# A fused attention and two-expert-layer kernel: identity transposes on TensorE while it waits, and its expert loops aligned to a fetch block

## The chip, the cores and the metric

The kernel runs on one core of one Trainium2 chip. The metric is the device time of one execution in microseconds (us); lower is better. Nothing is shared with other cores.

## What is computed

Three stages follow each other. A linear recurrence with a complex decay (4 batches, 8 heads, 768 steps, head size 48) gives 3072 rows of 384 numbers. A first expert layer sends every row to one of 8 experts (384 to 1024 to 384, with a ReLU between) and scales it by a gate. A second one does the same for the rows whose skip score is positive, and adds the result to them.

```
for t in range(S):
    new_re = ar * S_re - ai * S_im
    new_im = ar * S_im + ai * S_re
    S_re, S_im = (new_re + kv, new_im)
    y[:, :, t] = einsum('bhd,bhde->bhe', q[:, :, t], S_re)
...
expert_idx = argmax(logits, axis=1)
for e in range(E):
    mask = expert_idx == e
    h = maximum(x[mask] @ w1[e], 0.0)
    out[mask] = gate_w[mask, None] * (h @ w2[e])
```

## The kernel before

The recurrence is worked in 6 blocks c of 128 steps for 4 batches b, 24 steps n in all. For each block the logarithms of the decay are summed over its 128 steps by a matmul with a triangle of ones (`log_sum`, L1576, source tile `lm`), and its angles likewise (`angle_sum`, L1588 for block 0, source tile `an`). Exponentials of the first sums (tiles `ep` and `em`, ScalarE) and sines of the second (`kk`, `turn`, `cs`) are multiplied into q and k; TensorE transposes the products (L1619), and scores (L1633), state (L1650) and outputs (L1667, L1668) follow.

Both expert layers m = 0 and 1 share code. Rows are sorted by expert with a list in DRAM: GpSimd writes row numbers to it, reads the numbers of a tile back (`members`, L595, tile `idx_g`, semaphore `s_list[m]`) and gathers the rows with four indirect DMAs (`gather`, L602, tile `xg`, semaphore `s_xg[m]`). A tile s has up to 512 rows of one expert. On TensorE `rows_in` (L1776) transposes the tile, ScalarE and VectorE split it into a high and a low part (`xh` L930, `xl` L1359), `up` does 72 matmuls (L1788 to L1790), `down_a` or `down_b` the second product (L1805 to L1807, L1821 to L1823) and `results` L1835. `up` begins when `xl` is complete.

The tile count `used` and the length class of each tile (`code`, two bits a tile, looked up by `by_length`) are known at run time only. So each engine runs an outer loop over s in steps of 2, with an inner loop over the two halves, and each part of a tile's work stands four times, once for each length, behind compares and branches. `rows_in` for tile s + 1 stands inside the body of tile s, between the first part of the second product and its rest. Synchronisation is by semaphores written out by hand; the order on each engine is the order of the code. TensorE's instructions are written once in the order in which they run, apart from these branches; every matmul in the listings below is a weight load and a matmul, two instructions (four where the operands are plain float32 and it is no transpose, which runs in two passes).

Of the kernel before, what the change touches and what calls it, by code (L numbers as in the profile page):

```python
# [22 lines left out]
P = 128  # L23
# [4 lines left out]
def build(nc, H, a, qk, v, emb, tau, w1_a, w2_a, w_skip, w_gate, w1_b, w2_b, out):  # L28
    B, S, HD = v.shape
    D = HD // H  # L30
    C = S // P
    E, _, F = w1_a.shape
    N = B * S
    NT = N // P
    NS = N // 512 + E - 1
# [26 lines left out]
    with keep:  # L62
        def tensors(stack):
            return lambda name, shape, dt=F32: stack.enter_context(nc.sbuf_tensor(name, shape, dt))

        def sem(name):
            return keep.enter_context(nc.semaphore(name))
# [7 lines left out]
        ident = const("ident", [P, P])  # L75
# [74 lines left out]
        t_ = tensors(att)  # L150
# [34 lines left out]
        t_ = tensors(moe)  # L185
# [17 lines left out]
        T = [bank[0], bank[1]]  # L203
# [6 lines left out]
        DN = [bank[3], bank[4]]  # L210
# [13 lines left out]
        s_lm = sem("s_lm")  # L224
# [57 lines left out]
        def layer(name):  # L282
            return [sem(f"{name}_{m}") for m in range(2)]
# [12 lines left out]
        s_list = layer("s_list")  # L296
# [53 lines left out]
        def sum_bank(c, b):  # L350

            return (PL, PT[0], PT[1], PY)[b] if c == 0 else PL
# [1204 lines left out]
        def _(pe):  # L1557
            t = nc.tensor
# [8 lines left out]
            def log_sum(c, b):  # L1567

                n = B * c + b
                to = sum_bank(c, b)[:, 0:HD]  # L1570
                if c:
                    pe.wait_ge(s_exp, n)
                if b == 0 and c in (1, 2):
                    pe.wait_ge(s_turn, n)
                pe.wait_ge(s_logs, b // 2 + 1 if c == 0 else 2 * c + 2)
                t.matmul(to, tri_half[:, :], lm[:, b, :], start=True, stop=True).then_inc(s_L, 1)  # L1576

            def angle_sum(c, b):

                n = B * c + b  # L1580
                to = turn_bank(c, b)[:, 0:HD]
                if c == 0:
                    if b == 1:
                        pe.wait_ge(s_exp, 1)
                    if b == 3:
                        pe.wait_ge(s_turn, 1)
                    pe.wait_ge(s_angle, b // 2 + 1)
                    t.matmul(to, tri_turn[:, :], an[:, b, :], start=True, stop=True).then_inc(s_TH, 1)  # L1588
                else:
                    pe.wait_ge(s_turn, n - 1 if c == 1 and b > 1 else B * c if c == 1 else n)  # L1590
                    if c == 1 and b == 1:
                        pe.wait_ge(s_exp, 2 * B)
                    if c == 1:
                        pe.wait_ge(s_angle, 2 * c + 2)
                        t.matmul(to, tri_turn[:, :], an[:, b, :], start=True, stop=False)
                        t.matmul(to, last_row[:, :], turn[:, b, :], start=False, stop=True).then_inc(s_TH, 1)
                    else:
                        pe.wait_ge(s_carry, c - 1)
                        t.matmul(to, tri_turn[:, :], an[:, b, :], start=True, stop=True).then_inc(s_TH, 1)

            def sums(c, b):

                log_sum(c, b)
                angle_sum(c, b)
# [87 lines left out]
            def step(n):  # L1692
# [42 lines left out]
                if second and b == 0:  # L1735
                    sums(c + 1, 1)

            for b in range(B):
                log_sum(0, b)
            for b in range(B):  # L1740
                angle_sum(0, b)
            for n in range(2):
# [11 lines left out]
            for m in range(2):  # L1754
                tab = tab_of[m]

                def tiles(n):
                    return [(j, min(P, n - j * P)) for j in range((n + P - 1) // P)]

                def by_length(s, part):  # L1760
                    for i, n in enumerate(SIZES[m]):
                        with pe.If(((code >> (s * 2)) & 3) == i):
                            part(n)

                def rows_in(s, par):

                    pe.wait_ge(s_xg[m], s * 64 + 64)
                    if not isinstance(s, int):
                        pe.wait_ge(s_hl[m], FC * s)

                    def parts(n):
                        for side in (0,) if isinstance(s, int) else (0, 1):
                            with pe.If(par == side):
                                for k_ in range(KC):
                                    for j, w in tiles(n):
                                        i = t.transpose(U[k_][:, j * P:j * P + w], xg[0:w, side, j, k_ * P:(k_ + 1) * P], ident[0:w, 0:w])  # L1776
                                    i.then_inc(s_xT[m], 1)
                    by_length(s, parts)
# [59 lines left out]
                def rank_next(s):  # L1838

                    four = [P, TJ, E]  # L1840
                    to = QR.rearrange("p (t e) -> p t e", e=E)
                    pe.wait_ge(s_ohb, s + 1)
                    pe.wait_ge(s_sumb, s + 1)
                    t.matmul(to, before_t[:, :], oh_b[:, :, :], start=True, stop=False)
                    for j in range(1, TJ):
                        t.matmul(to[:, j:TJ, :], minus[:, :], oh_b[:, 0:TJ - j, :], start=False, stop=False)
                    t.matmul(to, minus[:, :], sum_b[:, :].unsqueeze(1).to_broadcast(four), start=False, stop=False)
                    t.matmul(to, minus[:, :], starts[:, :].unsqueeze(1).to_broadcast(four), start=False, stop=True).then_inc(s_rankb, 1)

                def count_next():  # L1850
                    for j in range(TJ):
                        t.matmul(QC, minus[:, :], oh_b[:, j, :], start=j == 0, stop=False)
                    t.matmul(QC, minus[:, :], sum_b[:, :], start=False, stop=True).then_inc(s_count, 1)

                def main(s, par):

                    pe.wait_ge(s_w1l[m], s + 1)
                    pe.wait_ge(s_xl[m], KC * s + KC)
                    by_length(s, lambda n: up(s, n))
                    if m == 0:  # L1860
                        with pe.If(s > 0):
                            rank_next(s - 1)
                        by_length(s, lambda n: down_a(s, n, (0,)))
                    else:
                        down_b(s, 0, P, False)
                    with pe.If(used > s + 1):
                        rows_in(s + 1, 1 - par)
                    if m == 0:
                        def rest(n):
                            down_a(s, n, (1, 2))  # L1870
                            results(s, n)
                    else:
                        def rest(n):
                            for j, w in tiles(n)[1:]:
                                down_b(s, j, w, j == tiles(n)[-1][0])
                    by_length(s, rest)
# [3 lines left out]
                pe.wait_ge(s_tab, m + 1)  # L1880
                used = pe.value_load(tab[0:1, USED:USED + 1], min_val=E, max_val=NS)
                code = pe.snap(pe.value_load(tab[0:1, CODE:CODE + 1], min_val=0, max_val=16383) + (pe.value_load(tab[0:1, CODE + 1:CODE + 2], min_val=0, max_val=16383) << 14))
                rows_in(0, 0)
                with pe.Fori(0, NS + 1, 2) as t_:
                    with pe.Fori(0, 2) as par:
                        s = t_ + par
                        with pe.If(used > s):
                            main(s, par)
                        if m == 0:
                            with pe.If(used == s):  # L1890
                                rank_next(s - 1)
                                count_next()
# [24 lines left out]
```

## Time and profile before

| | |
|---|---|
| times of the runs shown | 799.91, 801.9, 809.33 us; median 801.9 us |
| profiled execution | 801.38 us, its span 799.8 us |
| TensorE busy with matmuls | 663.7 us, 83% of the span |
| VectorE, ScalarE, GpSimd busy | 495.0, 406.6, 281.9 us |
| mean granted TensorE clock | 0.922 of full |

The span is from the first to the last instruction of the profiled execution; 1.6 us of that execution's time lie around it. The granted clock is 1.00 for 2.4 GHz and 0.50 for 1.2 GHz; in a stretch with both it is the mean. The attention stage lasts to about 312 us, the first expert layer from 330 to 600 us, the second from 626 us to the end.

### The profile page before, as it was taken

What the parts mean: (1) busy time and instruction counts of PE and PEld (TensorE: products, weight loads), DVE (VectorE), ACT (ScalarE), POOL (GpSimd) and SP (SyncE); (2) the same over time, 40 slices, a digit from 0 to 9 for tenths busy, and PEclk for the clock granted to TensorE, in tenths of its full rate; (3) what the DMA queues carried; (4) which work ended last, traced back from release to release, by engine and by line L of the source; (5) the groups of instructions that cost most, each with busy time, mean ns of one, the idle gap of its engine ahead of it and who ended that gap; (6) DMA issues with size and microseconds to landing.
All of it is one profiled execution on the core that took longest, in us unless ns stands there. A gap on an engine that the chain in (4) does not pass through costs nothing.

```text
span 799.8 us, 15830 instructions
## 1 busy us (share of the span) xinstructions
PE 663.7 (83%) x4754; PEld 608.9 (76%) x4754; DVE 495.0 (62%) x1169; ACT 406.6 (51%) x747; POOL 281.9 (35%) x315
## 2 busy tenths in 40 slices
PE   0678878998989993389999999999980689999993
PEld 0377767888878883378998999999870589999992
DVE  5564684977888665164755746757535366677770
ACT  7675586786685631162634635545421345455550
POOL 4304113142333232504335354262115425255531
PEclk9889789997999996599999999999995699999997
DMA  7431441524132520424335334353221255555630
GB/s 263 123 124 47 120 160 41 161 82 134 68 84 81 167 96 22 141 83 139 88 131 187 103 133 142 110 195 110 78 79 40 99 181 185 176 202 183 204 100 20
DMA packets 68580, 97.61 MB, mean 122 GB/s; under 512 B 28194, under 2 KB 51244, under 8 KB 68524
## 3 DMA queue, kind: packets, MB, share of 16 engines
q1 hardware_dynamic: 58028, 82.06, 31.8%
q0 software_dynamic: 10496, 14.84, 5.7%
q8 instruction: 30, 0.49, 0.2%
q14 instruction: 26, 0.21, 0.1%
HBM read 86.79 MB, written 21.04 MB: 135 GB/s over the span
## 4 chain that ended last, share of the span: by engine, by line
PE 70%; DVE 9%; ACT 8%; issue 8%; DMA 3%; POOL 1%; POOLq 0%; SPq 0%; DVEq 0%; ACTq 0%
PE bank L1788 8%; PE bank L1790 8%; PE bank L1789 8%; PE bank L1805 5%; PE bank L1807 4%; PE bank L1806 4%; PE bank L1619 3%; PE bank L1821 3%; PE bank L1633 3%; PE bank L1823 3%; PE bank L1822 3%; PE bank L1835 3%; PE bank L1650 3%; PE bank L1576 2%; PE bank L1776 2%
## 5 line engine op out<-in xcount | busy, mean ns | idle before, releaser
L1788 PE MATMUL bank<-xh,w1h 128*128 128x256 f32 (+3 forms) x384 | 124.7, 325 | 11.8 <-issue 5.7
L938 ACT ACTIVATE hh<-bank 128x256 fp32r<-128x256 f32 (+3 forms) x128 | 57.7, 451 | 135.6 <-PE bank L1790 135.3
L1789 PE MATMUL bank<-xh,w1l 128*128 128x256 f32 (+3 forms) x384 | 123.1, 321 | 0.0
L1790 PE MATMUL bank<-xl,w1h 128*128 128x256 f32 (+3 forms) x384 | 123.1, 320 | 0.0
L1367 DVE SCALAR_TENSOR_TENSOR hl<-bank,hh 128x256 fp32r<-128x256 f32 (+3 forms) x128 | 64.9, 507 | 61.1 <-ACT hh L938 53.6
L620 POOL DMA_INDIRECT out<-yg,idx_o x64 | 68.8, 1075 | 80.0 <-DVE yg L1428 47.7
L1788 PEld LDWEIGHTS bank<-xh,w1h 128*128 128x128 f32 x384 | 74.4, 194 | 16.9 <-issue 15.8
L1789 PEld LDWEIGHTS bank<-xh,w1l 128*128 128x128 f32 x384 | 74.3, 194 | 1.0
L1790 PEld LDWEIGHTS bank<-xl,w1h 128*128 128x128 f32 x384 | 74.2, 193 | 1.1
L1200 DVE TENSOR_TENSOR w2l<-raw,w2h 128x384 fp32r<-128x384 f32 x128 | 71.0, 555 | 0.0
L548 POOL TENSOR_TENSOR qk_t<-qk_t,ep 128x384 f32<-128x384 f32 x24 | 25.6, 1067 | 128.3 <-ACT em L750 101.5
L1805 PE MATMUL bank<-hh,w2h 128*128 128x384 f32 (+1 forms) x192 | 68.4, 356 | 1.5 <-issue 1.2
L1807 PE MATMUL bank<-hl,w2h 128*128 128x384 f32 (+1 forms) x192 | 67.1, 349 | 0.0
L1806 PE MATMUL bank<-hh,w2l 128*128 128x384 f32 (+1 forms) x192 | 67.0, 349 | 0.0
L631 POOL DMA_INDIRECT list<-pay,idx_b x32 | 37.0, 1156 | 83.3 <-DVE pay L1496 61.4
L801 ACT ACTIVATE w2h<-raw 128x384 fp32r<-128x384 f32 x128 | 66.2, 517 | 0.0
L1200 DVE TENSOR_TENSOR w1l<-raw,w1h 128x1024 fp32r<-128x1024 f32 x48 | 58.4, 1223 | 8.4 <-issue 6.6
L1776 PE MATMUL bank<-ident,xg 128*128 128x128 f32 (+1 forms) x132 | 21.3, 294 | 48.0 <-DMA xg<-out,idx_g 26.3
L602 POOL DMA_INDIRECT xg<-out,idx_g x32 | 33.6, 1051 | 71.2 <-DVE yg L1450 51.6
L556 POOL DMA_INDIRECT list<-token,idx_a x24 | 25.3, 1053 | 94.5 <-DVE idx_a L1178 77.4
L1776 PEld LDWEIGHTS bank<-ident,xg 128*128 128x128 f32 (+1 forms) x132 | 16.7, 150 | 51.7 <-issue 50.7
L930 ACT ACTIVATE xh<-bank 128x256 fp32r<-128x256 f32 (+3 forms) x48 | 19.5, 451 | 71.7 <-PE bank L1776 70.4
(230 smaller groups left out, 1655.0 us busy)
## 6 DMA issues: line engine op xcount, KB each, us to landing
raw<-in_moe_w SPq DMA_DIRECT2D x32, 1536.0 KB, 7.0
a_t<-in_a SPq DMA_DIRECT2D x24, 384.0 KB, 4.8
qk_t<-in_qk SPq DMA_DIRECT2D x24, 384.0 KB, 3.4
x_a<-ysb SPq DMA_DIRECT2D x24, 196.0 KB, 1.9
vt<-in_v SPq DMA_DIRECT2D x24, 192.0 KB, 3.5
list<-nobody SPq DMA_DIRECT2D x2, 1536.0 KB, 8.4
out<-yg,idx_o POOLq DMA_INDIRECT x64, 2.6
xg<-x_a,idx_g POOLq DMA_INDIRECT x32, 5.5
```

The source lines that it names most:

```text
L620: g.indirect_dma_start(out, bass.IndirectOffsetOnAxis(idx_o[:, par, j:j + 1], 0), yg[:, par, j, :], None, bounds_check=N - 1, oob_is_err=F ...
L801: return a_.activation(hi[:, at], raw[:, at], ACT.Copy)
L938: a_.activation(hh[:, f, 0:n], U[f % 3][:, 0:n], ACT.Relu).then_inc(s_hh[m], 1)
L1200: return d.tensor_tensor(lo[:, at], raw[:, at], hi[:, at].bitcast(F32), ALU.subtract)
L1367: d.scalar_tensor_tensor(out=hl[:, f, 0:n], in0=U[f % 3][:, 0:n], scalar=0.0, in1=hh[:, f, 0:n].bitcast(F32), op0=ALU.max, op1=ALU.subtrac ...
L1776: i = t.transpose(U[k_][:, j * P:j * P + w], xg[0:w, side, j, k_ * P:(k_ + 1) * P], ident[0:w, 0:w])
L1788: t.matmul(U[f % 3][:, 0:n], wh, xh[:, k_, 0:n], start=k_ == 0, stop=False)
L1789: t.matmul(U[f % 3][:, 0:n], wl, xh[:, k_, 0:n], start=False, stop=False)
L1790: i = t.matmul(U[f % 3][:, 0:n], wh, xl[:, k_, 0:n], start=False, stop=k_ == KC - 1)
L1805: t.matmul(DN[d_ % 2][:, 0:n], wh, hh[:, f, 0:n], start=f == 0, stop=False)
L1806: t.matmul(DN[d_ % 2][:, 0:n], wl, hh[:, f, 0:n], start=False, stop=False)
L1807: i = t.matmul(DN[d_ % 2][:, 0:n], wh, hl[:, f, 0:n], start=False, stop=f == FC - 1)
```

## The change

A helper `keep_busy(to, count)` issues `count` transposes of the 128x128 identity into the first 128 columns of a PSUM bank that nothing reads at that time. It is called with 14 behind a new wait on `s_lm` (VectorE's first step for the logarithms of batches 0 and 1 of block 0 is done), ahead of the first `log_sum`; with 12 ahead of the first `angle_sum`; and in each expert layer with 36 behind a new wait on `s_list[m]`, ahead of the first `rows_in`, and with 8 behind it. None of them raises a semaphore. And the outer loop of TensorE in both layers is written with `head_slot` 0: the instructions are fetched in blocks of 256, and the loop's first instruction is put at the first slot of such a block, with a jump over the slots left free ahead of it.

```diff
+            def keep_busy(to, count):
+
+                for _ in range(count):
+                    t.transpose(to[:, 0:P], ident[:, :], ident[:, :])
+
+            pe.wait_ge(s_lm, 1)
+            keep_busy(T[1], 14)
             for b in range(B):
                 log_sum(0, b)
+            keep_busy(T[1], 12)
             for b in range(B):
                 angle_sum(0, b)
...
+                pe.wait_ge(s_list[m], 16)
+                keep_busy(DN[0], 36)
                 rows_in(0, 0)
-                with pe.Fori(0, NS + 1, 2) as t_:
+                keep_busy(DN[0], 8)
+                with nc.Fori(0, NS + 1, 2, engines=(mybir.EngineType.PE,), head_slot={mybir.EngineType.PE: 0}) as t_:
                     with pe.Fori(0, 2) as par:
```

On TensorE, at the start of the program, before (each row is an operation with its line, its operands, its size and what it waits for):

```order
L1564 MATMUL bank<-ident,emb_q 112x8 x3
L1576 MATMUL bank<-lm,tri_half 128x384 [waits s_logs] x4
L1588 MATMUL bank<-an,tri_turn 128x384 [waits s_angle]
L1588 MATMUL bank<-an,tri_turn 128x384 [waits s_angle,s_exp]
L1588 MATMUL bank<-an,tri_turn 128x384 [waits s_angle]
```

And now:

```order
L1564 MATMUL bank<-ident,emb_q 112x8 x3
L1741 MATMUL bank<-ident 128x128 [waits s_lm]
L1741 MATMUL bank<-ident 128x128 x13
L1576 MATMUL bank<-lm,tri_half 128x384 [waits s_logs] x4
L1741 MATMUL bank<-ident 128x128 x12
L1588 MATMUL bank<-an,tri_turn 128x384 [waits s_angle]
```

The transposes (L1741) stand ahead of the first log sum and of the first angle sum; the waits of both are unchanged.

On TensorE, at the entry of expert layer 0, the last rows ahead of the loop and its first ones, before (L1762 is the lookup of the length, L1884 and L1885 the heads of the two loops):

```order
L1776 MATMUL bank<-ident,xg 128x128 x12
L1773 UNCONDITIONAL_BRANCH
L1884 UNCONDITIONAL_BRANCH
L1885 UNCONDITIONAL_BRANCH
L1885 ISA
L1887 COMPARE_AND_BRANCH
L1857 REGISTER_ALU
L1858 ISA [waits s_w1l_0]
L1762 REGISTER_ALU [waits s_xl_0]
```

And now, where L1784 is what L1776 was, and L1895 and L1896 are the loop heads:

```order
L1784 MATMUL bank<-ident,xg 128x128 x12
L1781 UNCONDITIONAL_BRANCH
L1741 MATMUL bank<-ident 128x128 x8
L1895 ISA
L1895 UNCONDITIONAL_BRANCH
L1896 UNCONDITIONAL_BRANCH
L1896 ISA
L1898 COMPARE_AND_BRANCH
L1865 REGISTER_ALU
L1866 ISA [waits s_w1l_0]
L1770 REGISTER_ALU [waits s_xl_0]
```

Eight transposes and the alignment (the first L1895 ISA) came between the tile's own transposes and the loop. The lines after the first insertion are 8 higher in the new kernel, those after the second 11.

## Rows read from the trace of the kernel before

**Rows 1.** The page: busy time by engine, and the chain that ended last by engine.
```profile
PE 663.7 (83%) x4754; PEld 608.9 (76%) x4754; DVE 495.0 (62%) x1169; ACT 406.6 (51%) x747; POOL 281.9 (35%) x315
...
PE 70%; DVE 9%; ACT 8%; issue 8%; DMA 3%; POOL 1%; POOLq 0%; SPq 0%; DVEq 0%; ACTq 0%
```

**Rows 2.** The view of waits, TensorE: us in total, times, longest.
```profile
PE bank L1776 <- DMA xg<-out,idx_g: 26.3, 1, 26.3
PE bank L1776 <- DMA xg<-x_a,idx_g: 18.7, 1, 18.7
```

**Rows 3.** The view of windows: stretch, length, busy time and operations, granted clock.
```profile
27.70:33.30 5.60, 5.49 (x8) 2.52 (x8) 3.70 (x7) 2.91 (x7) 2.46 (x3) 0.50 0.31 2
33.80:40.30 6.50, 4.06 (x32) 3.29 (x33) 6.36 (x10) 4.65 (x10) 0.00 (x0) 0.99 0.41 110
...
334.60:337.60 3.00, 2.96 (x9) 2.97 (x10) 0.00 (x0) 0.00 (x0) 2.20 (x3) 0.50 0.50 139
337.60:348.60 11.00, 11.00 (x64) 11.00 (x64) 6.94 (x14) 6.35 (x14) 1.61 (x2) 1.00 0.10 22
358.10:361.50 3.40, 3.40 (x12) 3.33 (x12) 2.89 (x7) 3.04 (x6) 2.04 (x2) 0.51 0.16 30
...
629.20:634.50 5.30, 5.29 (x25) 5.30 (x26) 1.61 (x4) 1.59 (x4) 4.38 (x5) 0.50 0.17 41
634.50:640.40 5.90, 5.90 (x49) 5.77 (x48) 4.77 (x11) 3.98 (x10) 0.09 (x1) 0.99 0.05 3
```

**Rows 4.** The timeline of TensorE, sums: start, us, line, form, count, idle before.
```profile
19.78 4.76 PE L1576 MATMUL bank<-lm,tri_half 128*128 128x384 f32 x8 [12.13 <-DVE lm L1070]
27.77 5.49 PE L1588 MATMUL bank<-an,tri_turn 128*128 128x384 f32 x8 [3.24 <-ACT an L741]
...
59.63 0.89 PE L1576 MATMUL bank<-lm,tri_half 128*128 128x384 f32 x2 [1.05 <-DVE lm L1070]
```

**Rows 5.** The timeline of VectorE and ScalarE at the start.
```profile
15.30 1.83 DVE L1057 SCALAR_TENSOR_TENSOR lm<-lr,w 128x768 f32<-128x768 f32 x2 [1.64 <-ACT w L719]
...
21.47 0.49 ACT L749 ACTIVATE ep<-bank 128x384 f32<-128x384 f32 x1 [2.00 <-PE bank L1576]
...
25.59 1.28 ACT L797 ACT_TABLE_LOAD   x1
...
29.46 0.56 DVE L1081 TENSOR_SCALAR kk<-bank 128x384 f32<-128x384 f32 x1 [8.86 <-PE bank L1588]
```

**Rows 6.** The chain of waits, in order of time: the lists and the second layer's entry.
```profile
317.27 2.31 DMA idx_g<-list
...
616.62 2.37 DMA idx_g<-list
...
626.32 0.70 PE bank L1776 x2
...
628.31 0.44 DVE xl L1359
628.75 0.46 issue
629.21 0.57 PE bank L1788
...
641.35 0.55 DVE w2l L1200
```

**Rows 7.** The timeline of TensorE in expert layer 0.
```profile
330.48 2.17 PE L1776 MATMUL bank<-ident,xg 128*128 128x128 f32 x9 [18.67 <-DMA xg<-x_a,idx_g]
...
353.40 0.43 PE L1776 MATMUL bank<-ident,xg 128*128 128x128 f32 x2 [0.44 <-issue]
356.47 1.84 PE L1776 MATMUL bank<-ident,xg 128*128 128x128 f32 x10 [2.64 <-issue]
...
391.85 1.14 PE L1776 MATMUL bank<-ident,xg 128*128 128x128 f32 x9
```

**Rows 8.** The page, DMA queues: packets, MB, share.
```profile
q8 instruction: 30, 0.49, 0.2%
```

## The prediction

> **What bounds the kernel now.** I read the page first: TensorE is busy for 83% of the span and makes 70% of the chain that ended last [rows 1]. So most of the 801.4 us is matmul time, and none of the added transposes can remove a matmul. What can be removed is time in which matmuls run at half clock and time in which TensorE idles without a partner to wait for. The view of waits shows the two long idle stretches, 18.7 us ahead of the first layer's rows and 26.3 us ahead of the second's [rows 2]. Both are chains of GpSimd and DMA, which the change doesn't touch. The windows show what they leave behind: the granted clock is 0.50 for the first 3.0 us of matmuls in layer 0 and for the first 5.3 us in layer 1, and 1.00 and 0.99 right behind [rows 3]. The reader is to see that the same operations take twice the time there: 9 matmuls in 2.96 us against 64 in 11.00, so 0.33 against 0.17 us, and 25 in 5.29 against 49 in 5.90, so 0.212 against 0.120. The third such place is the start: the angle sums run wholly at 0.50 [rows 3], 1.69 us from their first pass to the first `kk` that reads one (27.77 to 29.46), and the log sums show the same 1.69 us (19.78 to 21.47) [rows 4, 5], where two passes later in the program take 0.89 [rows 4]. Last, TensorE idles for 2.64 us in the middle of the twelve transposes of tile 1, in layer 0's first pass through the loop, and the releaser is "issue": nothing in the profile was waited for [rows 7]. At 358.10 the clock is at 0.51 again for 3.4 us [rows 3].
>
> **The change, part by part.** A transpose of 128x128 costs 2.17 us for nine at half clock and 1.14 for nine at full [rows 7]; without the tail of the last one that is about 0.21 and 0.11 us each.
>
> *14 transposes ahead of the log sums.* `s_lm` rises when the first of the two steps at 15.30 is done, about 16.2 us [rows 5]. They take 14 x 0.21 = 3.0 us and end at 19.3, ahead of the log sums at 19.78: no delay, with 0.4 us to spare. Does the clock rise in time? The traces bound it: it rose 3.0 us after the first matmul of layer 0 and 7 us after the transposes ahead of it, 5.3 and 8.2 us in layer 1, and about 6 us after the angle sums began [rows 3, 4, 6, 7]. From 16.2 that is 19.2 to 24.4 us, so during the log sums as likely as ahead of them. If ahead, the first exponential starts 0.8 us sooner (1.69 less 0.89), and the eight of them, 0.49 each, need 3.9 us in place of 4.1 (21.47 to the table load at 25.59 [rows 5]): 1.0 us. If late, nothing. I take 0.6.
>
> *12 transposes ahead of the angle sums.* They fill 1.4 of the idle 3.24 us [rows 4]; nobody waits for them. If the clock holds, the angle sums give 0.8 us; if it falls in the 2.5 us still idle, 0. I take 0.4. Their rest is hidden: from the second `kk` on VectorE is busy with its own chain. First stage together: 1.0 us, ends 0 and 1.8. It carries on, since TensorE's and VectorE's work from there on is one chain and the loads are ahead.
>
> *36 transposes and the new wait in layer 0.* The numbers of the rows have landed at 319.6 [rows 6]; 36 transposes take 4 to 7.7 us and end by 327.3. Queued behind the wait is only `rows_in`, which waits until 330.48 anyway [rows 7]. But 3 to 6 us of idle time follow, as long as the idle 3.24 us at whose end the angle sums found half clock [rows 3, 4]. So I expect the clock to be down again for `rows_in`, and these 36 to bring nothing here.
>
> *8 transposes behind `rows_in`, layer 0.* 17 transposes in a row from 330.48 last until about 334.1, just short of the first matmul at 334.6. The work is now unbroken from 330.48, so the clock should rise at about the time when the matmuls begin, and not 3 us later: 9 x 0.16 = 1.4 us. Ends: 0, and 2.4 with the nine transposes at full clock too (1.0 less). I take 1.3.
>
> *The same in layer 1.* The list lands at 618.99 [rows 6] and the tile's transposes start at 626.32, 7.3 us later. 36 transposes fill it: if the clock rises 3 to 6 us in, they end at 624 to 626, and the idle gap behind them is short. So here the clock should be up at once: 25 x (0.212 - 0.120) = 2.3 us, and 0.2 from the tile's first two transposes (the three `xl` on VectorE hide the rest). The end of the up part is followed by the last `hh`, `hl` and `w2l` (to 641.9 us) [rows 6], which move with it. 2.5 us, if nothing else is late.
>
> *The alignment.* In the code, 1005 instructions lie between the loop's head and the place where TensorE stops in layer 0, behind two transposes and the weight load of a third. I read this stop as a block of instructions that isn't there yet; the queue that carries instructions moved 30 packets, 0.49 MB, so 16 KB each [rows 8]. With blocks of 256, 1005 = 1024 - 19: the head stands 19 slots into a block now, and with head slot 0 the border moves 19 instructions down, to exactly behind this tile's twelve transposes. If the block comes no sooner, ten transposes (10 x 0.11 us) run ahead of the stop and not behind it: 1.0 us. Ends: 0, and 2.64 + 1.7 (the half-clock stretch at 358.10, which the stop explains) if the block is there in time. Against this, the jump over the free slots: ahead of layer 0 there are 10 us of waiting to hide it. Ahead of layer 1 I count the wait for the rows and the loop's head two blocks apart, so that the block between is entered only once the rows are there, at about 626.9, and the head is touched some 0.6 us behind that. A stop of 2.64 us as in layer 0 then lasts from 627.6 to 630.2, and with the 0.46 us between `xl` and the first matmul this starts at 630.7, not 629.21 [rows 6]: minus 1.5 us. Ends: 0 and minus 4.
>
> The page "Runtime: NRT & Kernel Launch" of the Trainium skill, section "Instruction fetch mechanics", says that instructions come in 16 KiB blocks of 256, that blocks are prefetched in sequence, and that a taken branch to a block that isn't there forces a fetch first. The packet size agrees with the first; the stop stands in straight code, which the last alone wouldn't give.
>
> **Sum.** 1.0 + 1.3 + 1.0 + 2.5 - 1.5 = 4.3 us. The profiled execution took 801.38 us, 0.5 below the median shown; 801.4 - 4.3 = **797.1 us**.
>
> **Rivals.**
>
> *Transposes don't wake the clock.* Then only the alignment is left, and the 36 transposes in layer 1 end at 619.0 + 7.7 = 626.7, 0.4 us late, and the eight behind `rows_in` at 629.7, still hidden by the missing head. 1.0 - 1.5 gives 801.9 us. For it: in both layers the clock was still at half after the tile's transposes. Against it: from 33.8 to 40.3 us TensorE ran nothing but transposes, 4.06 busy of 6.50, and the clock held at 0.99 [rows 3]. The Trainium skill's page "TensorE: Matmul & The Clock Gate", Part 4, states this rule (transposes don't count as busy time in the same way); by this row the trace speaks against it, at least for holding the clock.
>
> *More idle time, not less: slower.* The mechanism is that work which got faster leaves a gap in which the clock falls. At the start, angle sums at full clock end some 3 us sooner while the first q and k products come only 1.8 sooner, so the idle time ahead of L1619 grows from 1.4 to about 3 us; then the 32 transposes and 32 score passes run at half clock, about 3 us more on the chain, against 1.8 won. In layer 1 the missing head leaves 2.8 us idle and the 2.5 us are lost too. With layer 0 won only by its alignment: 1.2 + 1.5 - 1.0, 803 us. It decides once a gap reaches about 3.2 us, the one that was seen to cost the clock [rows 4]. For it: both gaps come out just under that.
>
> *All of it comes.* Clock up at all three places (1.8 + 2.4 + 2.5), the stop gone with its half clock (4.3), the head in time: 11.0 us, 790.4 us.
>
> *The loop no longer fits.* If moved blocks made each tile's pass miss one, 16 passes x 2.64 = 42 us, 844 us. Against it: the stop stands once in the trace, and from slot 0 the loop of 1673 instructions touches no more blocks than from 19.
>
> **How the numbers follow.** My forecast has a chance of 0.55, the transposes without effect 0.12, the new gaps 0.13, all of it 0.16, the missing blocks 0.04. From 790.5 to 803.5 us the range holds the first four with the bounds of their parts; three times of the same kernel spread over 9.4 us, which is more than the forecast gain. 2%, 16 us, is about what a measurement of this kernel tells from no change. Faster by more than that would need more than everything above: 0.01. Slower: the missing blocks, 0.04. The rest, 0.95, is no change.
>
> **What would show each step.** In the profile after: first `ep` 0.8 us sooner and `kk` nearly 2; the transposes at 0.21 us changing to 0.11 within the 36; a clock of 1.00 in the first 5 us of matmuls in layer 1; twelve unbroken transposes and a stop behind them in layer 0; an "issue" gap of about 1.5 us more between `xl` and L1796 in layer 1. I am wrong if the first matmuls of layer 1 still run at 0.212 us, if stops stand in later passes, or if the attention stage, whose idle gaps all move, gets other stretches of half clock than it had.

## The result, and the profile after

The changed kernel takes 794.2 us (median of 20 runs, 786.6 to 802.9), the kernel before 800.4 us on the same chip (20 runs, 794.1 to 809.3). The ratio is 0.990, interval 0.987 to 0.993: 8 us or 1% faster. Every ratio of this study is taken without the runs that lie more than 1.5% above the fastest of their kernel; over all runs the two medians differ by 6.3 us. On two other chips the same kernel gave 0.9873 [0.983, 0.992] and 0.9899 [0.985, 0.995]. The forecast of 797.1 us had the direction and held the time in its range, and its 4.3 us were two thirds of the difference of the medians and half of what the ratio gives.

The profiled execution of after is one of its long ones, 800.8 us with a span of 799.2, so the two spans (799.8 before) show nearly no gain. The stages do. Each time below is the difference of two starts in the timeline of TensorE; "up" is the first matmul of the first product of an expert (L1788 before, L1796 after), "rows" the first transpose of a tile.

| stage | before | after | difference |
|---|---|---|---|
| first `lm` (L1057) to first q transposes (L1619) | 19.35 | 17.42 | -1.9 |
| attention, L1619 to the last count matmul | 276.99 | 280.27 | +3.3 |
| to the rows of layer 0, and on to its first up | 23.00 | 23.57 | +0.6 |
| first pass of the loop, layer 0 (up to up) | 37.1 | 33.1 | -4.0 |
| rows of layer 1 to its first up | 2.89 | 4.77 | +1.9 |

The first `lm` started 0.7 us earlier (14.61 against 15.30), which makes up the rest. So the change gains 5.9 us at two places, loses 1.9 at a third, and attention took 3.3 us more in this one execution. The timeline of TensorE at the start (start, us, line, form, count, idle before):

```profile
15.62 3.25 PE L1741 MATMUL bank<-ident 128*128 128x128 f32 x14 [7.96 <-DVE lm L1057]
19.09 3.22 PE L1576 MATMUL bank<-lm,tri_half 128*128 128x384 f32 x8 [0.22 <-DVE lm L1070]
22.14 1.47 PE L1741 MATMUL bank<-ident 128*128 128x128 f32 x12
25.79 4.54 PE L1588 MATMUL bank<-an,tri_turn 128*128 128x384 f32 x8 [2.17 <-ACT an L741]
32.03 1.08 PE L1619 MATMUL bank<-ident,qcs 128*96 128x128 f32 x8 [1.70 <-DVE kcs L1106]
```

Against [rows 4], the eight log sums take 3.22 us and not 4.76, the angle sums 4.54 and not 5.49: full speed for a part of each. The 14 transposes took 0.23 us each, the 12 behind the log sums 0.12. So the speed rose between them, during the log sums. Counted from the first `lm`, the first `ep` comes 0.4 us sooner than before, the table load 1.3, the first `kk` 2.0 (20.41, 23.60 and 26.74 less 14.61, against [rows 5]):

```profile
14.61 1.83 DVE L1057 SCALAR_TENSOR_TENSOR lm<-lr,w 128x768 f32<-128x768 f32 x2 [1.64 <-ACT w L719]
...
26.74 0.56 DVE L1081 TENSOR_SCALAR kk<-bank 128x384 f32<-128x384 f32 x1 [6.84 <-PE bank L1588]
```
```profile
20.41 0.49 ACT L749 ACTIVATE ep<-bank 128x384 f32<-128x384 f32 x1 [1.63 <-PE bank L1576]
...
23.60 1.28 ACT L797 ACT_TABLE_LOAD   x1
```

The view of the first fence again, at layer 0:

```profile
320.68 5.58 PE L1741 MATMUL bank<-ident 128*128 128x128 f32 x36 [8.22 <-DMA idx_g<-list]
331.74 2.17 PE L1784 MATMUL bank<-ident,xg 128*128 128x128 f32 x9 [5.48 <-DMA xg<-x_a,idx_g]
333.71 1.91 PE L1741 MATMUL bank<-ident 128*128 128x128 f32 x8
335.86 0.68 PE L1796 MATMUL bank<-xh,w1h 128*128 128x384 f32 x1 [0.24 <-issue]
...
353.64 2.10 PE L1784 MATMUL bank<-ident,xg 128*128 128x128 f32 x12 [0.19 <-issue]
356.96 0.43 PE L1813 MATMUL bank<-hh,w2h 128*128 128x384 f32 x1 [1.22 <-issue]
...
368.93 0.46 PE L1796 MATMUL bank<-xh,w1h 128*128 128x448 f32 x1 [1.28 <-issue]
```

The 36 transposes need 5.58 us where half clock alone would need 7.7 (36 at the prediction's 0.21 us), so the clock rose inside them; 5.48 idle us later the tile's nine are at half clock again. The stop of 2.64 us amid tile 1's transposes [rows 7] is gone: all twelve run in a row, and 1.22 us of stop stand behind them. And at layer 1:

```profile
616.49 6.14 PE L1741 MATMUL bank<-ident 128*128 128x128 f32 x36 [19.05 <-DMA idx_g<-list]
623.60 0.87 PE L1784 MATMUL bank<-ident,xg 128*128 128x128 f32 x6 [0.97 <-DMA xg<-out,idx_g]
624.53 1.09 PE L1741 MATMUL bank<-ident 128*128 128x128 f32 x8
628.36 0.57 PE L1796 MATMUL bank<-xh,w1h 128*128 128x256 f32 x1 [2.74 <-issue]
```

Here the transposes of the tile run at full clock, the last `xl` ends at 625.6, and then TensorE stands 2.74 us for nothing that the profile shows, where it was 0.46 before [rows 6]. The windows (length, busy time and operations of the five engines, granted clock, share and GB/s of the DMA engines) show what the clock did:

```profile
331.00:334.60 3.60, 2.86 (x14) 2.87 (x15) 1.24 (x3) 1.48 (x3) 0.00 (x0) 0.50 0.02 5
334.60:337.30 2.70, 2.46 (x10) 2.07 (x8) 0.43 (x1) 0.00 (x0) 2.03 (x2) 0.50 0.28 68
337.30:348.00 10.70, 10.70 (x63) 10.70 (x63) 6.14 (x12) 5.67 (x13) 2.81 (x3) 1.00 0.18 45
356.00:360.00 4.00, 3.04 (x17) 3.05 (x18) 3.59 (x7) 2.72 (x5) 2.80 (x3) 1.00 0.42 134
617.00:625.00 8.00, 6.96 (x45) 6.49 (x44) 0.52 (x2) 0.94 (x3) 4.87 (x5) 0.77 0.59 226
625.00:627.40 2.40, 0.63 (x6) 0.39 (x4) 0.57 (x2) 0.00 (x0) 1.79 (x2) 1.00 0.14 29
627.40:634.20 6.80, 5.84 (x27) 5.85 (x28) 1.95 (x4) 1.60 (x4) 3.05 (x4) 0.50 0.11 22
```

In layer 0 half clock ends 1.4 us into the matmuls (3.1 before), and it doesn't come back behind the second tile's transposes, where [rows 3] had 0.51. In layer 1 it is up until 627.4 and gone just before the matmuls, which then run at half clock for their first 5.9 us (to 634.3), as they did before for 5.3.

### The profile page after: what moved, and what is told of

The parts are those of the page before. It is cut to its first block, busy times and chain, and to the rows that moved or that the text cites. A ratio compares the mean times of both kernels' runs of the same rounds, so it can differ in the third digit from the quotient of the medians.

```text
span 799.2 us, 16060 instructions
## 1 busy us (share of the span) xinstructions
PE 680.7 (85%) x4868; PEld 624.2 (78%) x4868; DVE 494.7 (62%) x1169; ACT 406.3 (51%) x747; POOL 280.0 (35%) x315
## 4 chain that ended last, share of the span: by engine, by line
PE 67%; ACT 9%; DVE 9%; issue 8%; DMA 3%; POOL 2%; POOLq 0%; SPq 0%; DVEq 0%; ACTq 0%
PE bank L1796 8%; PE bank L1797 8%; PE bank L1798 8%; PE bank L1813 5%; PE bank L1814 4%; PE bank L1815 4%; PE bank L1829 3%; PE bank L1831 3%; PE bank L1830 3%; PE bank L1619 3%; PE bank L1843 3%; PE bank L1650 3%; PE bank L1633 2%; PE bank L1784 2%; PE bank L1667 2%
## 5 line engine op out<-in xcount | busy, mean ns | idle before, releaser
L1796 PE MATMUL bank<-xh,w1h 128*128 128x256 f32 (+3 forms) x384 | 124.5, 324 | 11.5 <-issue 8.8
L1796 PEld LDWEIGHTS bank<-xh,w1h 128*128 128x128 f32 x384 | 74.2, 193 | 16.4 <-issue 15.4
L1813 PE MATMUL bank<-hh,w2h 128*128 128x384 f32 (+1 forms) x192 | 67.7, 352 | 2.6 <-issue 2.3
L1633 PE MATMUL bank<-qT,kT 96*128 96x128 f32 x384 | 51.7, 291 | 2.5 <-ACT kT L768 2.4
L1633 PEld LDWEIGHTS bank<-qT,kT 96*128 96x128 f32 x384 | 47.8, 202 | 3.5 <-ACT kT L768 2.7
```

The costliest lines, as they stand in the source:

```text
L1633: i = t.matmul(PT[j][:, (h % 4) * P:(h % 4 + 1) * P], kT[:, n % 2, h * P:(h + 1) * P], qT[:, n % 2, h * P:(h + 1) * P], start=True, stop=True)
L1796: t.matmul(U[f % 3][:, 0:n], wh, xh[:, k_, 0:n], start=k_ == 0, stop=False)
L1813: t.matmul(DN[d_ % 2][:, 0:n], wh, hh[:, f, 0:n], start=f == 0, stop=False)
```

## The experiments

Twelve timings of ten kernels on three chips, each beside the kernel before, which took 817.1, 802.7 and 815.8 us there; ratios are to it.

**One part at a time: the loops' alignment.** The kernel before, with the loops' heads put at slot 0:

```
-  with pe.Fori(0, NS + 1, 2) as t_:
+  with nc.Fori(0, NS + 1, 2, engines=(mybir.EngineType.PE,), head_slot={mybir.EngineType.PE: 0}) as t_:
```

> The kernel before with head slot 0 on both TensorE loops and no added transposes. Theory 1: the stop of 2.64 us moves from the middle of tile 1's twelve transposes to behind them (12 in one row, then 1.2 to 1.6 us of issue idle), gain 1.0 us, with 1.7 more if the clock doesn't fall there; in layer 1 the missing head costs about 1.5 us. Together within 1.5 us of the kernel before, 799 to 802 us. Rival (the alignment is what makes the changed kernel faster): 792 to 795 us, as the changed kernel.

Ratio 0.9998 [0.996, 1.004]: nothing. The trace shows both sides of it. The twelve transposes run unbroken, with 1.36 us of stop behind them and no half clock there; but a new stop comes ahead of the first matmul of layer 0:

```profile
339.39 0.68 PE L1788 MATMUL bank<-xh,w1h 128*128 128x384 f32 x1 [3.46 <-issue]
...
357.94 2.11 PE L1776 MATMUL bank<-ident,xg 128*128 128x128 f32 x12 [0.30 <-issue]
361.41 0.43 PE L1805 MATMUL bank<-hh,w2h 128*128 128x384 f32 x1 [1.36 <-issue]
```

Rows to first up is 5.6 us (4.2 before), the first pass 34.1 (37.1). Alignment alone takes the stop out of the loop and puts one at its door. In after, with the transposes in front, the idle time at the door of layer 0 is 0.24 us. The 1.5 us that the expectation gave to layer 1 did not come: rows to first up is 2.89 us there, as before, with no stop.

**The transposes without the alignment.** After, with the plain loops of before:

> The changed kernel with all 70 transposes and plain loops, so that the code ahead pushes layer 0's head to slot 159 by my count and its 1673 instructions touch 8 blocks instead of 7. Theory 1 (8 blocks still fit, only first passes miss): about as fast as the changed kernel, 792 to 797 us, the stops of layer 0's first pass elsewhere, and layer 1 without the 2.74 us ahead of its first matmul. Rival (with 8 blocks each pass pushes one out and fetches it again, 2.6 us a time): 8 tiles x 2.6 or more, 815 us and up, and far more than 32 packets on the instruction queue.

908.3 us, ratio 1.107 [1.101, 1.114]. The page (queue of instructions: packets, MB, share) and the view of waits (us in total, times, longest):

```profile
q8 instruction: 96, 1.57, 0.8%
```
```profile
PE bank L1796 <- issue: 66.3, 11, 10.9
...
PE bank L1813 <- issue: 17.6, 8, 3.4
```

96 packets of 16 KB where every other kernel of the study moved 30 to 33, 84 us of idle time with no releaser ahead of L1796 and L1813 (6.9 us ahead of the same two lines, L1788 and L1805, before), and layer 0's loop takes 368 us and not 265. The rival in the expectation came true. By the count of the code, the added instructions push this loop's head from slot 19 of a block of 256 to slot 159. Its 1673 instructions end in slot 1692 from 19, within seven blocks (1792), and in slot 1832 from 159, in an eighth. From slot 0 or 64 it is seven. So the alignment shows no gain by itself and is what makes the rest possible: the forecast's rival of a loop that no longer fits is real, and the change's own alignment excludes it. The rival was priced at 2.64 us a pass, 42 us; the stops ahead of L1796 alone are 5.8 to 10.9 us a pass, and it costs 91 us against the kernel before and 100 against the change.

**Layer 1's door.** Its head moved to slot 64, so that the block with the head is entered before the wait:

```
-  head_slot={mybir.EngineType.PE: 0}
+  head_slot={mybir.EngineType.PE: 64 * m}
```

> The changed kernel, with the loop head of layer 1 at slot 64 of its block instead of slot 0 (layer 0 stays at 0). By my count the code ahead of layer 1's loop ends at slot 58, so the jump goes over 6 free slots and stays in its block, where slot 0 made it jump to a block not yet entered. Theory 1 (the 2.74 us of issue idle between the eight transposes and L1796 is the missing block of the loop head): the gap shrinks to about 1 us, the first matmuls of layer 1 run at full clock (0.12 us each, not 0.21), and the kernel is 1.5 to 4 us faster than the changed one. Rival (the gap is the sequencer's own work, compares and branches behind the transposes): gap and time stay as they are.

Beside it on the same chip ran the change once more:

> The changed kernel once more, on the same chip as the three others, for a second profile of it. 0.99 of the kernel before, 792 to 796 us. Theory 1 for the profile: the layer 1 gap of 2.7 us stands again, while the clock at its end may be full or half, since the clock's falls sit at other places in each execution. Rival: the gap was a chance of the one profile and is gone.

The change has the stop at the door again, and its up part at full clock nevertheless; with slot 64 the stop is gone from there, and two others stand ahead of the down part and ahead of the second tile's up part. First the change, then slot 64:

```profile
629.32 0.38 PE L1796 MATMUL bank<-xh,w1h 128*128 128x256 f32 x1 [3.17 <-issue]
```
```profile
627.22 0.38 PE L1796 MATMUL bank<-xh,w1h 128*128 128x256 f32 x1 [0.41 <-DVE xl L1359]
...
639.32 0.41 PE L1829 MATMUL bank<-w2h,hh 128*128 128x384 f32 x1 [2.54 <-issue]
...
651.87 0.41 PE L1796 MATMUL bank<-xh,w1h 128*128 128x256 f32 x1 [2.90 <-issue]
```

Ratio 0.9925 [0.988, 0.997] against 0.9873 [0.983, 0.992]: no better, and the expected 1.5 to 4 us did not come. From the rows of layer 1 to the second tile's first up it is 27.1 us with slot 64 and 25.5 in the change beside it. The slot doesn't remove the stop; it moves it, and here it made two of it.

**Start and layers apart.** The start's 26 transposes alone, with the loops' heads kept where they were (slots 19 and 0), and the change without these 26:

```
+  pe.wait_ge(s_lm, 1)
+  keep_busy(T[1], 14)
...
+  keep_busy(T[1], 12)
...
+  head_slot={mybir.EngineType.PE: 19 * (1 - m)}
```

> The kernel before with the 14 and 12 transposes at the start alone; the loops are held where they were, at slot 19 in layer 0 and slot 0 in layer 1 by my count. Theory 1: the first transposes of q and k (L1619) come 1.9 us sooner, and this stays: 0.997 to 0.999 of the kernel before. Rival (the start shifts where the clock falls in the whole attention stage, and most of the 8 us of the change come from there): 0.992 or less.

> The changed kernel without the 14 and 12 transposes at the start: 36 and 8 in each layer and both loops at slot 0. Theory 1: layer 0's first matmuls find the clock up 1 to 3 us sooner, layer 1's find it up at once where it doesn't fall in the 2.7 us gap; together 3 to 5 us, 0.994 to 0.997. Rival (the start brings the most): 0.998 to 1.0.

Ratios 0.9972 [0.994, 1.001] and 0.9963 [0.992, 1.000]: 2.3 and 3.0 us, together 5.2 with some 4 of uncertainty, against 8.4 us for the change over three chips (by the ratios, weighted by the number of runs). Neither part is clear of no change by itself, and over all runs their medians differ from before by only 0.4 and 1.6 us. The traces are sharper. The start is 2.0 us shorter with the 26 transposes (17.32), and 19.22 without. Layer 0's first pass is 39.5 us in the first, with the stop amid the transposes (3.53 us), and 32.6 in the second. The first kernel isn't wholly the kernel before in layer 0: it reaches its head at slot 19 by a jump, and has a stop at that door too, which before had not:

```profile
337.94 0.68 PE L1796 MATMUL bank<-xh,w1h 128*128 128x384 f32 x1 [2.38 <-issue]
...
360.70 1.65 PE L1784 MATMUL bank<-ident,xg 128*128 128x128 f32 x7 [3.53 <-issue]
```

From the rows of layer 0 to its second up it takes 44.0 us where the kernel before took 41.3, so its timing may show the start for less than it is worth. Layer 1's door has 3.09 us of stop in the second:

```profile
634.67 0.57 PE L1793 MATMUL bank<-xh,w1h 128*128 128x256 f32 x1 [3.09 <-issue]
```

**A filler ahead of the list.** After, and 24 transposes between layer 0's loop and the wait for the table of layer 1:

```
+  else:
+      keep_busy(DN[0], 24)
```

> The changed kernel with 24 more identity transposes on TensorE between the loop of layer 0 and the wait for layer 1's table, so that by my count TensorE's wait for the first rows of layer 1 stands 11 slots into the block ahead of the loop head (with slot 0 kept), and that block is entered some 20 us before the rows. Theory 1 (the gap ahead of L1796 in layer 1 is the block of the loop head, asked for only when the block ahead of it is entered): the gap of 2.7 to 3.2 us becomes about 0.5, the stops of the first pass stay where they were, and the stretch from the first rows_in of layer 1 to its first L1829 falls from 15.4 us (18.0 where the clock had fallen in the gap) to about 13; the kernel is 2 to 4 us faster than the changed one. Rival (the jump over the free slots costs this by itself): the gap stays.

Ratio 0.984 [0.979, 0.989]. The stop at layer 1's door is gone, the clock is up, and nothing is late behind it. Rows to first up is 2.5 us, and rows to the first L1829 12.8, as expected:

```profile
623.15 0.87 PE L1784 MATMUL bank<-ident,xg 128*128 128x128 f32 x6 [2.00 <-DMA xg<-out,idx_g]
...
625.65 0.38 PE L1796 MATMUL bank<-xh,w1h 128*128 128x256 f32 x1 [0.57 <-DVE xl L1359]
```

The same, with 76 transposes ahead of layer 0's rows where the change has 36, so that they reach the rows:

> As filler, with 76 transposes in place of 36 ahead of layer 0's rows. In the changed kernel the 36 were followed by 4.5 to 5.5 us of idle time, and the clock was at half again for the tile's nine transposes and the first matmuls. 40 more fill 4.3 us of that. Theory 1 (the idle gap is what lets it fall): the nine transposes run at full clock, 1.1 us instead of 2.2, the first matmuls at 0.17 us each, and the kernel is 1.5 to 3 us faster than filler. Rival (the clock doesn't matter there, since xl on VectorE and the lookup set the first matmul): only the matmuls' 1 to 1.5 us, or nothing.

Ratio 0.9885 [0.984, 0.994], and on the third chip 0.9854 [0.978, 0.993] (expectation below). The nine transposes of the tile took 1.19 us and not 2.17, matmuls at full clock from the first:

```profile
308.83 10.12 PE L1741 MATMUL bank<-ident 128*128 128x128 f32 x76 [8.22 <-DMA idx_g<-list]
319.12 1.19 PE L1784 MATMUL bank<-ident,xg 128*128 128x128 f32 x9 [0.17 <-issue]
...
322.47 0.43 PE L1796 MATMUL bank<-xh,w1h 128*128 128x384 f32 x1 [1.28 <-DVE xl L1359]
```

but rows to first up is 3.3 us with either kernel. The first pass is 33.6 us (32.4 in the second trace) against 34.6 with the filler alone, and 33.1, 32.3 and 32.4 in the three traces of the change, so the traces show no gain by the longer row, and neither do the times.

**Attention's gaps.** The ten traces so far had attention stages of 268 to 284 us with 24 to 54 us of half clock in them. The last four timings ask whether the two are cause and effect: the change and the kernel above once more, and identity transposes in seven gaps of attention, as many as fit, and half as many.

```
@@ step n of attention; the counts of the second kernel are half of these
+  if n == 1: keep_busy(T[1], 10)   ahead of log_sum(1, 0)
+  if n == 2: keep_busy(T[1], 14)   ahead of angle_sum(1, 0)
+  if n == 5: keep_busy(T[1], 18)   ahead of sums(2, 0)
+  if n == 6: keep_busy(T[1], 18)   ahead of transposes(n + 2, 0)
+  if n == 0: keep_busy(PL, 26)     ahead of transposes(n + 2, 1)
+  if n == 4: keep_busy(PL, 12)     ahead of transposes(n + 2, 1)
+  keep_busy(T[1], 12)              ahead of the first transposes(0, 0)
```

> The change once more, on the chip of the next three, as their base. Both theories: ratio 0.987 to 0.993 to the kernel before, the stop ahead of the first up matmul of layer 1 at 2.7 to 3.2 us. Its attention stage (first transposes of the queries to the count matmul) took 280.3 and 276.3 us in the two traces so far, with 44 and 38 us of half clock in it.

> The change with 24 more transposes after the layer-0 loop and 76 instead of 36 ahead of it, once more. If its ratio of 0.9885 was a matter of the chip, it comes to 0.984 or lower here, as the kernel with the 24 alone did; if the longer row of transposes costs what it gives, 0.987 to 0.99. The attention stage is untouched by it: between 268 and 284 us, whatever the clock happens to do.

> As filled_again, and identity transposes also in seven gaps of 1.6 to 3.5 us that TensorE has in the first 140 us of attention (12, 26, 10, 14, 12, 18 and 18 of them, into banks that it holds at that time). Theory A, that the 24 to 54 us of half clock in the attention stage come from these gaps and cost about half their length (the stages of nine traces: 268.3 us at 23.9 us of half clock, 284.4 at 54.1): half clock only from 88 to 98 us, where one gap stays, and at the end, the stage at 262 to 270 us, 8 to 15 us less than the kernel filled: 778 to 786 us where the kernel before has 802. Theory B, that the attention stage is set by VectorE, ScalarE and GpSimd and the half clock only shows their stops: stage within 3 us of filled_again, ratio 0.984 to 0.99. Theory C, the transposes that run past the gap at half clock (26 of them take 3.9 us where the gap is 3.5) hold up the chain: stage 1 to 5 us longer.

> As attn_fill with half as many transposes in each of the seven gaps (6, 13, 5, 7, 6, 9, 9). Theory A: if half a gap filled is enough for the clock, the same 778 to 786 us; if not, between filled_again and attn_fill, 786 to 792. Theory B: as filled_again. Theory C: no cost of its own, since no row is longer than its gap at either clock.

| kernel | ratio | mean clock of its runs | attention in its trace, half clock in it |
|---|---|---|---|
| before | 1 | 0.921 | 277.0, 42 |
| the change | 0.9899 [0.985, 0.995] | 0.932 | 281.8, 52 |
| filled | 0.9854 [0.978, 0.993] | 0.941 | 272.7, 37 |
| seven gaps full | 0.9812 [0.975, 0.987] | 0.952 | 273.8, 22 |
| seven gaps half full | 0.9845 [0.980, 0.989] | 0.953 | 268.7, 18 |

The row before has the trace of the first chip, 277.0 us, beside the clock of the third. Theory A is half right. Half clock does come from the gaps: with them half full, two stretches are left between 31 and 105 us (51 to 55, and 85 to 96 where a gap stays open) where the change has five. The total in a single trace says less, since two of the traces without transposes in attention had 24 us of it too; the mean clock of the timed runs says it again, 0.952 and 0.953 against 0.941. The 8 to 15 us did not come: both kernels took 0.997 of the time of the kernel filled beside them (interval about 0.99 to 1.005), so no gain over it is shown. By the mean clock, the runs of the change show 0.44 us more span for each us more at half clock (20 runs, correlation 0.89). The mean clocks give some 19 us less of it with the gaps filled, which would be 8 us; six runs each don't show that so much came back, and hardly exclude it.

One place where the half clock does cost shows in the traces: the time between the state products (L1650) of successive steps. The timeline of TensorE, these products of steps 0 to 3, before and after:

```profile
44.20 1.48 PE L1650 MATMUL bank<-vt,kcs 128*96 128x48 f32 x16
...
60.35 1.48 PE L1650 MATMUL bank<-vt,kcs 128*96 128x48 f32 x16
...
73.85 1.48 PE L1650 MATMUL bank<-vt,kcs 128*96 128x48 f32 x16
...
90.86 2.69 PE L1650 MATMUL bank<-vt,kcs 128*96 128x48 f32 x16
```
```profile
42.24 1.48 PE L1650 MATMUL bank<-vt,kcs 128*96 128x48 f32 x16
...
58.70 2.68 PE L1650 MATMUL bank<-vt,kcs 128*96 128x48 f32 x16
...
75.13 2.69 PE L1650 MATMUL bank<-vt,kcs 128*96 128x48 f32 x16
...
95.08 2.69 PE L1650 MATMUL bank<-vt,kcs 128*96 128x48 f32 x16
```

Steps 1 and 2 take 13.5 and 17.0 us before, 16.4 and 19.9 after, where these products and what follows run at half clock for 6.8 us in each:

```profile
57.40:64.20 6.80, 6.80 (x34) 5.05 (x36) 3.29 (x5) 1.74 (x4) 2.21 (x3) 0.50 0.08 27
74.50:81.30 6.80, 6.80 (x30) 4.76 (x29) 3.52 (x7) 0.00 (x0) 0.85 (x1) 0.50 0.01 2
```

Of the twelve traces without transposes in attention five have the short pair and seven the long one, some 5.8 us apart, and none lies between: the short one before and with the alignment alone, the long one in all three traces of the change. Both kinds occur with the start's transposes and without. The attention stage is 273.5 us in the mean of the five and 280.0 in that of the seven, with single ones of either kind at 280.5 and 275.9. With half-full gaps the pair was 13.5 and 17.3, with full gaps 15.1 and 17.6.

## Why the forecast was right in direction and short in size

**Start: forecast 1.0 us, measured 1.9.** The step's bounds were 0 and 1.8, so this term was mis-sized, just beyond its upper end. All eleven traces with these transposes have 17.1 to 18.0 us from `lm` to the first q transposes, the three without 19.2 to 19.8. The speed rose during the first two log sums, so the first `ep` gained only 0.4 us, but the eight exponentials, which were fed one by one, then ended 1.3 us sooner where 0.6 was taken. The angle sums, priced at 0.4, gave the other 0.7: the 2.17 idle us ahead of them didn't lower the clock for the first one (0.95 us from its start to its `kk`, 1.69 before), and the half clock from 26.7 to 30.1 us fell on sums that VectorE wasn't waiting for.

**Layer 0: forecast 1.3 + 1.0, measured 4.0.** This is the step that was mis-sized most. What the 36 do was right (the clock is down again), and so was where the border lands, behind twelve transposes. But the forecast took the stop as unchanged at 2.64 us and left the half clock behind it in the range, as an end and not as the value. In the trace the stop is 1.22 us (1.4 less), and the half clock that followed it, 3.4 us of it at [rows 3], is gone (1.7 us at half speed). The entry's matmuls have 1.7 us less at half clock: 0.9, not 1.3. That makes 4.0, the measured 37.1 less 33.1. On the second chip it was 39.5 against 32.6, the first of them in the kernel that reaches slot 19 by a jump. That the shorter stop alone keeps the clock up is argued, not tried: in the kernel with only the alignment it was 1.36 us, and the clock stayed up there too. Why the stop is shorter behind the transposes than amid them no run shows.

The three kernels apart show what each part does here. From the rows of layer 0 to its second up it is 41.3 us before, 39.7 with the alignment alone, and 37.2, 36.4 and 35.9 in the three traces of the change. So the alignment gives 1.6 us net of the stop that it puts at the door, and the transposes, with which that stop doesn't show, another 2.5 to 3.8.

**Layer 1: forecast 2.5 - 1.5, measured -1.9.** The stop was forecast from the code at 1.5 us of delay. From the last `xl` to the first matmul it is 2.8 us in place of 0.46: 2.3 us, inside the bounds, of which the faster transposes of the tile take back 0.46. What fell is the independence of the two terms: the stop makes the gap in which the clock falls, so the 2.5 us didn't come in this execution. The prediction has this case among its rivals, the new gaps, and had named it as a sign of being wrong: the first matmuls of layer 1 run at 0.21 us again. In two other executions of the same kernel the clock survived 3.17 and 3.15 us of stop. In the first of them the stretch from layer 0's last pass to layer 1's second took 88.2 us, and 88.0 with the alignment alone on the same chip. On the second chip it was 90.9 us without the start's transposes, and 87.3 in the kernel with these alone, whose layer 1 is that of before. So the term is between a loss of 3.6 us and nothing. The filler shows it the other way round: without the stop this stretch is 85.8 us on that chip.

**The whole.** The forecast's 4.3 us are near the 1.9 + 4.0 - 1.9 = 4.0 us of the profiled pair, but by luck: two places gave more than forecast and the third had the wrong sign. Attention put 3.3 us against it, of which no term spoke; that it gets other stretches of half clock was the prediction's third sign of being wrong, and it came. With 6.9 for layer 0 and 0 for layer 1, as on the other chips, the sum is up to 8.8. The 8.4 us of the timed runs lie at the upper end. About 3 us between them and the parts timed apart (5.2) stay within the uncertainty of both; whether attention has a share in them is open, since the timed runs leave no trace of their stages, only their clock.

**The rivals.** That transposes don't wake the clock fell: in the layers it rose within 36 transposes of the identity, which took 5.58 and 6.14 us in after and 6.02 in the second trace of the change, with no matmul near. At the start the log sums, which ran 4.76 us at half speed before, sped up behind 14 of them. The page "TensorE: Matmul & The Clock Gate" of the Trainium skill, Part 4, says that transposes don't count as busy time in the same way; this case's traces don't bear that out. That new gaps let the clock fall was true in layer 1, and in attention in as far as the long pair of steps came with it in all three traces, though the one trace of the kernel before can't say that it came by it; both together didn't outweigh the rest. That all of it comes (790.4 us, 0.1 outside the range that was to hold it) fell with layer 1. The loop that doesn't fit is shown by the kernel without alignment, at 91 us against the forecast's 42.

## What to carry to other kernels

Idle time on TensorE can be paid twice where the engine is needed right behind it: the stop of 2.64 us in straight code cost its length and half of the 3.4 us at half clock that followed, so ask of each gap on the chain what the clock does behind it before pricing the gap alone. Transposes of the identity kept the clock up where they reached to the work. Behind a row that ended 5 us early the clock was down again, and behind one that was followed by a stop of some 3 us it was down in two traces of four. And whoever adds instructions ahead of a long loop should count its blocks: here 26 + 44 transposes without an alignment cost 11%.

The simplest version that goes beyond the change is the one with 24 transposes ahead of layer 1's table (0.984 [0.979, 0.989]), whose trace shows the stop gone; it was not timed beside the change on one chip, and the two intervals overlap. With half-full gaps in attention on top it had 0.9845 [0.980, 0.989] on another chip, so the step beyond the filler isn't shown to be one.

## What the runs showed of the hardware

A loop of 1673 instructions that lay in seven blocks of 256 ran with 30 to 33 instruction packets for the whole program, and in eight blocks with 96 packets and stops of up to 10.9 us. A stop in straight code moved with the border of its block and didn't vanish, but its length differed with the place: 2.64 and 3.53 us amid a tile's transposes, 0.7 to 1.4 behind them in the eleven traces with the head of layer 0 at slot 0. Two executions of one kernel had gaps of 2.74 and 3.17 us at the same place, and the clock fell in the shorter one and not in the longer. Attention ran with one of two patterns of half clock, some 5.8 us apart over two steps. And a reading of 1.00 can be no reading: at the start of the program the window says 1.00, and the 14 transposes take 0.23 us each, as at half clock, where the 12 a little later take 0.12:

```profile
15.60:19.00 3.40, 3.25 (x14) 2.85 (x14) 2.88 (x5) 3.15 (x4) 0.00 (x0) 1.00 0.89 280
```

The clock records of this trace begin at 19.9 us, so the 1.00 ahead of them is the absence of a record. They begin at 18.6 to 21.1 us in all eleven traces with the start's transposes and at 23.7 to 25.9 in the three without, which fits the first rise of the clock. So the speed ahead of it has to be read from the durations.
